# The experts' weight pieces fetched in two interleaved transfers each instead of one

## What is computed

```python
x = sliding_window_attention(q, k, v)            # window 64, 8 heads of 64
xn = x / rms(x) * rms_g                          # first MLP: 512 -> 1536 -> 512
x = (silu(xn @ w_gate) * (xn @ w_val)) @ w_out
noisy = x @ r_gate + log1p(exp(x @ r_noise)) * noise    # router, 8 experts
top2, weights = two largest of noisy, softmax over the two
out = sum over the two experts e of weight_e * (relu(x @ w1[e]) @ w2[e])
# w1[e] is 512 x 1024, w2[e] is 1024 x 512: 2 MB each, 4 MB an expert
```

## Time and profile before

| | us |
|---|---|
| median of 3 runs | 1099.86 (1099.44 to 1100.42) |
| profiled execution: its time | 1101.53 |
| its span | 1099.7 |
| PE busy | 1046.6 (95%) |
| PE weight loads busy | 905.8 (82%) |
| DVE busy | 640.1 (58%) |
| POOL busy | 386.6 (35%) |
| ACT busy | 328.6 (30%) |

### The profile page before, as it was taken

How to read it: one execution, slowest core, us unless ns; L and a number is a source line. 1 busy time by engine, 2 the same in 40 slices (tenths; PEclk the granted TensorE clock), 3 DMA queues, 4 the chain that set the end, 5 groups by cost and what they waited for, 6 DMA issues and landing times.

```text
span 1099.7 us, 19425 instructions
## 1 busy us (share of the span) xinstructions
PE 1046.6 (95%) x5749; PEld 905.8 (82%) x5749; DVE 640.1 (58%) x1302; ACT 328.6 (30%) x724; POOL 386.6 (35%) x358
## 2 busy tenths in 40 slices
PE   8999999999999999999999979989897999989976
PEld 7888999999999999999988768868685877768755
DVE  6886343463453453543576957667565766667654
ACT  7986222432432431523451030201102030200222
POOL 4667980030120300300558070523406070510485
PEclk9999999999999999999999999999898999999999
DMA  8985535311313214110467485766748585645897
GB/s 229 279 264 184 154 105 163 115 58 30 115 58 88 84 34 119 57 23 9 163 182 221 114 261 152 219 184 189 233 136 256 135 249 164 216 130 154 240 287 255
DMA packets 254382, 173.42 MB, mean 158 GB/s; under 512 B 134833, under 2 KB 206401, under 8 KB 254305
## 3 DMA queue, kind: packets, MB, share of 16 engines
q1 hardware_dynamic: 232448, 115.01, 36.8%
q10 hardware_dynamic: 16032, 38.47, 10.5%
q0 software_dynamic: 5824, 18.95, 5.0%
HBM read 105.79 MB, written 62.65 MB: 153 GB/s over the span
## 4 chain that ended last, share of the span: by engine, by line
PE 55%; SPq 18%; DMA 13%; issue 5%; DVE 5%; POOL 3%; ACT 0%; DVEq 0%; POOLq 0%
PE bank L904 27%; PE bank L936 14%; DMA hidden_by_blocks<-relu 9%; SPq L616 9%; SPq L581 6%; PE bank L1072 4%; PE bank L1093 3%; DMA hidden_blocks<-hidden_by_blocks 2%; PE bank L848 2%; SPq L586 2%; PE bank L875 2%; POOL token_rows_a L781 1%; DMA token_rows_b<-expert_rows,slots_u 1%; SPq L391 1%; PE bank L858 1%
## 5 line engine op out<-in xcount | busy, mean ns | idle before, releaser
L904 PE MATMUL bank<-x_parts,mlp_weights 128*128 128x384 f32 x1704 | 309.3, 336 | 0.0
L904 PEld LDWEIGHTS bank<-x_parts,mlp_weights 128*128 128x128 f32 x1704 | 298.2, 188 | 5.3
L1093 PE MATMUL bank<-expert_parts,hT_high 128*128 (+1 forms) x688 | 223.7, 407 | 40.4 <-DVE hT_low L1861 29.8
L1072 PE MATMUL bank<-expert_parts,xT_high 128*128 (+1 forms) x688 | 213.8, 392 | 0.0
L1093 PEld LDWEIGHTS bank<-expert_parts,hT_high 128*128 128x128 f32 x688 | 133.6, 196 | 76.9 <-issue 49.2
L763 POOL TENSOR_TENSOR expert_parts<-raw_expert_a,expert_parts 128x512 fp32r<-128x512 f32 x64 | 81.5, 1307 | 249.7 <-ACT expert_parts L1398 247.4
L936 PE MATMUL bank<-mlp_weights,hidden_parts 128*128 128x512 f32 x648 | 162.0, 394 | 0.0
L1072 PEld LDWEIGHTS bank<-expert_parts,xT_high 128*128 128x128 f32 x688 | 127.7, 188 | 29.1 <-issue 3.2
L936 PEld LDWEIGHTS bank<-mlp_weights,hidden_parts 128*128 128x128 f32 x648 | 120.2, 188 | 23.2 <-issue 1.0
L1093 PE MATMUL bank<-expert_parts,hT_low 128*128 (+1 forms) x344 | 138.5, 403 | 0.0
L1072 PE MATMUL bank<-expert_parts,xT_low 128*128 (+1 forms) x344 | 134.0, 390 | 0.0
(11 more groups left out here) (220 smaller groups left out, 1213.4 us busy)
## 6 DMA issues: line engine op xcount, KB each, us to landing
hidden_by_blocks<-relu SPq DMA_DIRECT2D x76, 256.0 KB
hidden_blocks<-hidden_by_blocks SPq DMA_DIRECT2D x304, 64.0 KB
raw_expert_a<-in_w ACTq DMA_DIRECT2D x32, 512.0 KB
raw_expert_b<-in_w ACTq DMA_DIRECT2D x32, 512.0 KB, 5.3
x_row<-routed_rows SPq DMA_DIRECT2D x172, 64.0 KB
expert_rows<-y_row SPq DMA_DIRECT2D x43, 256.0 KB
expert_rows<-zeros SPq DMA_DIRECT2D x4, 2304.0 KB, 11.9
v_sb<-in_v SPq DMA_DIRECT2D x32, 256.0 KB, 4.0
```

The lines of the kernel that those rows point to most:

```text
L904: last = nc.tensor.matmul(bank[:, 0:CHUNK], w_sb[:, i, wp, at:at + P], xp[:, par, part, k, :], start=n == 0, stop=n == 3 * KB - 1)
L1072: last = nc.tensor.matmul(ps[half][:, 0:512], (xTh, xTl)[xp][:, buf, k, :], ew_sb[:, bass.ds(slot, 1), wp, k * F2 + half * 512:k * F2 + ha ...
L1093: last = nc.tensor.matmul(y_bank(t)[:, 0:D], (hTh, hTl)[hp][:, f, :], ew_sb[:, bass.ds(slot, 1), 2 + wp, f * D:(f + 1) * D].rearrange("p a ...
```

## The change

Each piece comes in two transfers, which both raise the piece's semaphore by 16; the wait ahead of the high part asks for twice the count. For w1 the 4096 bytes of a partition are cut in eight runs of 512 bytes, of which one transfer takes the even and the other the odd ones. For w2 each row of 2048 bytes is cut in two runs of 1024, one for each transfer. Buffers, order and all other waits stay as they are.

```diff
-            if kind == 0:
-                src = w1_pieces[bass.ds(at, 1)].rearrange("e p f -> p (e f)")
-            else:
-                src = w2_pieces[bass.ds(at, 1)].rearrange("e p a d -> p (e a) d")
-                dst = dst.rearrange("p (a d) -> p a d", a=2)
-            act.dma_start(dst, src).then_inc(expert_in[q % 4], 16)
+
+            for odd in range(2):
+                if kind == 0:
+                    src = w1_pieces[bass.ds(at, 1)].rearrange("e p (j o n) -> p (e j) o n", o=2, n=P)[:, :, odd]
+                    to = dst.rearrange("p (j o n) -> p j o n", o=2, n=P)[:, :, odd]
+                else:
+                    src = w2_pieces[bass.ds(at, 1)].rearrange("e p a (o n) -> p (e a) o n", o=2)[:, :, odd]
+                    to = dst.rearrange("p (a o n) -> p a o n", a=2, o=2)[:, :, odd]
+                act.dma_start(to, src).then_inc(expert_in[q % 4], 16)
...
-            act.wait_ge(expert_in[q % 4], 64 * pair + 16 * (q // 4) + 16)
+            act.wait_ge(expert_in[q % 4], 128 * pair + 32 * (q // 4) + 32)
```

## The result

The changed kernel takes 1106.32 us, the median of 20 runs (1100.53 to 1111.75); the kernel before took 1100.32 us beside it (20 runs, 1094.31 to 1108.45). The ratio is 1.0046, with a 95% interval of 1.0025 to 1.0066: some 5 us slower, where 4.6 us faster were forecast. 1106.32 lies inside the range given, but the sign was wrong. (A ratio is taken from executions beside each other and is not the quotient of the two medians; in this document the two differ by up to 0.2%, 2 us.)

The account below looks back on a forecast made before the run. PE, busy 95%, bounds the kernel and loses 38.4 us in six stretches with weight transfers, where SP's store is late. +5.9 - 12.5 + 2 = -4.6 us from 1099.9 gives 1095 us; range 1084 to 1110.

Parts of the forecast that it names:

- part 1: Weight transfers of experts 2 to 7: smaller packets add 9.8 us of engine time, costing +5.9 us (+0.8 to +12).
- part 2: Stretches with weights: SP's transfers stand behind blocks about 0.5 us shorter, giving -12.5 us (0 to -16.7).
- part 3: ACT's added issues, uncovered only in the four w1 loads before L1311 in the MLP's last chunk: +2 us (+1.1 to +2.8).
- part 4: Later landing of each piece's second half: hidden by four raw buffers and early arrival, or by the MLP's last blocks; no term.
- the slack of 0.36 us: MLP's last chunk: DVE's low part ends at 539.66, PE takes L936 at 540.02; 0.36 us to absorb added issues.
- slower rival: SP's last pending transfer waits behind both halves, so part 2 is 0: 1108 us, upper bound some 1113; chance 0.35.

Follow-up runs that it names:

- steady_only: Kernel before, with the change's two transfers a piece for experts 2 to 7 alone: 1103.57 us, ratio 0.9979 to the kernel before.
- eight_big: Kernel before, with pieces of experts 2 to 7 in eight transfers of 512 bytes a partition over all partitions: 1091.75 us, ratio 0.9903.
- half_parts: Kernel before, with pieces of experts 2 to 7 in two transfers of 64 partitions each, whole rows: 1116.67 us, ratio 1.0133.
- extra_issue: Kernel before, with an added transfer of 32 bytes a partition into an unused buffer after each piece of experts 2 to 7: 1101.11 us, ratio 1.0006.
- w1_big_w2_small: Kernel before, with experts 2 to 7's w1 in halves of 2048 contiguous bytes, w2 in the change's 1024-byte halves: 1097.25 us, ratio 0.9974.

## Why the prediction was wrong, step by step

| step | forecast | what the runs showed |
|---|---|---|
| part 1, engine time | +9.8 us, worth +5.9 | +6.5 us of engine time; its worth of 0.6 each not shown by any run |
| part 2, shorter turns | -12.5 (0 to -16.7) | with part 1 -2.3 (two kernels: 0.9979, 0.9977) |
| part 3, ACT's issues | +2 (+1.1 to +2.8) | +5.2 alone; 7.6 for the first four pieces; 7.0 in the trace |
| part 4, landing | 0 | PE waits once for GpSimd's parts, 4.5 us (3.7 before) |

**The failed step is part 3**: its term was +2 us and measured 5 to 8, some 3 to 6 us more. Parts 1 and 2 together were too good by 4.3 us; either miss alone would have left the kernel about level, and both made it slower. The place was foretold (the burst of four ahead of L1311, PE at L936 near 540) and so was the slack of 0.36 us. Four things in the sum were wrong.

First, the value taken from its own range. The burst's issues, after and before:

```profile
L1385 ACTq DMA_DIRECT2D raw_expert_a<-in_w x4: 551/557/672, 534.5 to 538.2; - x4
L1385 ACTq DMA_DIRECT2D raw_expert_b<-in_w x4: 550/551/625, 539.5 to 542.4; - x4
```

```profile
L1382 ACTq DMA_DIRECT2D raw_expert_a<-in_w x2: 349/354/359, 533.9 to 535.2; - x2
L1382 ACTq DMA_DIRECT2D raw_expert_b<-in_w x2: 339/339/339, 537.0 to 538.1; - x2
```

An issue of 512 runs took 0.55 to 0.67 us, as the row of L581 had it (0.58). Both halves of a piece have 512 runs, so the upper bound of 0.78 us a piece was the one to take, but +2 lay in the middle of the range. All eight issues last 4.61 us and the four of before 1.39, so (4.61 - 1.39) / 4 = 0.81 us a piece was measured.

Second, an issue is more than its own time. The eight issues are 4.61 of the 8.45 us, the four of before 1.39 of 4.53. Between two pieces ACT reads the expert's number from a table (L391):

```profile
L391 ACTq TENSOR_LOAD <-tab x4: 325/472/1067, 533.0 to 537.4; - x4
```

and ahead of each second issue stand 0.16 us of register instructions. So four pieces took 8.45 - 4.53 = 3.92 us more, 0.98 each: 3.92 - 0.36 = 3.56 us is the wait seen, 3.48. The pair of loads in the earlier trace rows, 1.43 us for two issues of 0.34, showed that time between them.

Third, I counted a wait of PE at its own length, though part 2 of the same sum had put 1.5 on idle time for the clock; here it was 1.7 us on 3.5.

Last, I looked at the burst and not at the pieces of w2 in the blocks behind it, with which it gave the second wait of 1.64 us.

**Part 2 had the right sign and was oversized.** Part 1 and part 2 were to give -6.6 us together, and gave -2.3 (uncertain by 2). Plain halves of the same size without the smallest packets gave -5.3 in the mean, so even then 0.66 us off a turn was worth about 8 us per us, not the 25 (12.5 / 0.5) that I put down. SP's waits for the store did not fall (54.0 us). That fits the slower rival, by which the last of several pending transfers still stands behind both halves; that it does, no run shows. The rival's result, slower by engine time in this stage, did not come about: steady_only is 2.3 us faster. That 1106.32 lies near the rival's 1108 us is chance.

**Part 1's sizes were right, its price is open.** The packets last 28 and 45 ns. eight_big has 16.3 us more engine time, which at 0.6 would cost 9.8 us, and is the fastest of all: the price, if there is one, is outweighed there. For a price speaks half_parts, +14.6 us with 23.8 us more engine time; against it speak extra_issue, +0.7 us with 7.7, and w1_big_w2_small, which without the packets of 512 bytes was hardly faster than the change's halves (2.9 and 2.3 us). The 3 us between the change's halves and plain ones would fit it (6.5 x 0.6 = 3.9), but no run tests it alone.

By the Trainium skill, "DMA: Bandwidth & Descriptors", section "Rules for kernel authors", many small transfers are best joined into a large one. At the start the runs agree: with the first pieces in one transfer each the kernel is 5 to 8 us faster. Beside SP's store and read-back, a case of which that rule doesn't speak, they disagree: 64 KB transfers in place of 512 KB ones gained 10.7 us. The measurement decides, and it is the place that matters.

Open stay: why the first four pieces split alone cost 10 us in the median where experts 0 and 1 split whole cost 5; how much of the gain of four and eight transfers is the turn and how much the spacing; and what the strided halves pay that plain ones don't.

## What to carry to other kernels

An edit to a transfer in a loop is also an edit to its first burst: price each added issue there by a row with as many runs, add the register instructions ahead of it, subtract the slack once, and give the wait of PE its clock as well. Split a long transfer only where the engine that issues it has time, and leave the first ones whole. Where another queue's short transfers set the pace, as here, cut into plain blocks over all partitions, and try quarters or eighths before halves.

## What was unexpected in the hardware

- Transfers over 64 partitions kept their engines busy for longer per packet: 12.5% x 16 x 1114.0 us / 16800 = 133 ns in the mean for queue 10, against 10.5% x 16 x 1099.7 / 16032 = 115 ns before, where three quarters of the pieces were cut. In transfers over 32 partitions the engine time was 133.1 us, near eight_big's 131.8, and the kernel some 13 us slower than that one. By the Trainium skill, "DMA: Bandwidth & Descriptors", section "Rules for kernel authors", two transfers to disjoint halves of the partitions aren't worth it because they serialize; here they were worse than that, 1.3% slower than one.
- An issue on ACT takes longer with more runs: 0.55 us with 512 runs, 0.40 with 256, 0.34 to 0.35 with 128 (medians). Four loads in a row took 4.53 us, of which the issues themselves were 1.39.
- Eight transfers of 512 bytes a partition in place of one of 4096 made this kernel faster by 0.97%, with 12.1% instead of 10.5% of the DMA engines' time on that queue.
